# A 256-column moving operand read as interleaved 16-column runs

## The chip, the cores and the metric

One NeuronCore of a Trainium2 chip runs the kernel. The metric is the device time of one execution in microseconds (us), lower is better. A NeuronCore has five engines that run their own instruction streams and meet at semaphores: TensorE (PE in the profile; its weight loads are listed as PEld), VectorE (DVE), ScalarE (ACT), GpSimd (POOL) and SyncE (SP). Here SP and POOL only start transfers, apart from a few constants that POOL writes at the start.

## The reference

Attention of 8x8 heads over a small state, then two feed-forward blocks over 4608 tokens. The second feed-forward block is the part that the change touches.

```python
def _attn_ref(x, state):            # x (8, 8, 512, 64), state (8, 8, 32, 64)
    ...                             # two softmaxes, xread and sread
    return np.concatenate([xread, sread], axis=2)

def _moe_ref(x, w_in, w_out):       # 4608 tokens, 512 -> 2048 -> 512
    h = np.maximum(x @ w_in, 0.0)
    return h * h @ w_out

def _moe2_ref(x, w1, w2, w3, w_out):    # 4608 tokens, 512 -> 1024 -> 1024 -> 512
    a = x @ w1
    b = x @ w2
    h = a * b @ w3
    return h @ w_out

def reference(**kwargs):
    attn_out = _attn_ref(...)
    x = attn_out.transpose(0, 2, 1, 3).reshape(4608, 512)
    x = _moe_ref(x, ...)
    return _moe2_ref(x, ...)
```

## The kernel before

**Number format.** Every matrix product is made of float32r operands: each float32 value is held as a rounded high part and the rest as a low part, and a product takes three matmuls, high by high, high by low, low by high. The helper `product` (line 658) issues them. It is the helper's line 661 that the profile names for nearly every matmul. In `nc.tensor.matmul(dst, w, m)` the second argument is the stationary operand (the weights, 128 columns, loaded by a weight load of its own before each matmul), the third is the moving operand, whose columns are streamed through the array. The profile prints a matmul as `dst<-moving,stationary`.

**Stages.** Up to about 100 us, tables are built (`w3` times `moe2_w_out`, the state times `w_in`). Then follow the eight batches of 512 tokens, with attention woven in, through the first feed-forward block (matmuls with 512 moving columns), and a ninth, short block of 256 tokens (moving columns 256, from some 680 us on). At 720.92 us the second feed-forward block begins, called stage 2 here. It lasts to the end.

**Stage 2.** The products `x @ w1` and `x @ w2` are not made directly. For each pair of token tiles (halves of the 512 tokens of a batch) and the two matrices, a Strassen-Winograd scheme takes seven products of sums in place of eight. The seven sums on the side of the weights, S_hi and S_lo, lie in rows of several tensors (`E_hi`, `E_lo`, `top`, `aT_hi`, `X_hi` and others, hence the many names in the profile). The seven sums on the side of the tokens are `B_hi[:, j, kk]` and `B_lo[:, j, kk]`, j = 0 to 6, kk = 0, 1 for the two halves of the inner dimension, each 256 columns wide. They are views into the tensors `X_hi` and `X_lo`, which start `SHIFT = 80` columns (320 bytes) into them:

```python
        B_hi, B_lo = (t[:, 0:N_SETS + 1].rearrange("p k n -> p (k n)")[:, SHIFT:SHIFT + N_SETS * C]
                      .rearrange("p (j k n) -> p j k n", j=N_SETS, k=2) for t in (X_hi, X_lo))
```

In the built program every stationary operand of the kernel starts 128 bytes past a multiple of 512 bytes within its partition, and so does every moving operand, but for these block sums: they start 448 bytes past one, which is the 320 bytes of SHIFT further.

The engines' programs of stage 2 are written out by hand, in chunks. For batch t and output chunk m (0 to 7):

- `ab_chunk(t, m)` on TensorE: seven products of two halves and three passes, 42 matmuls of 256 moving columns, into four banks of `ps_h` and `ps_t`. It starts when VectorE is done with the banks of the chunk before (`ab_done`), at m = 0 it waits for each new set of token sums (`set_ready`), and the fifth product waits until ScalarE has copied the first (`P1_copied`).
- `out_chunk(t, m - 1)` on TensorE: four output tiles by three passes, 12 matmuls of 512 moving columns, from `v_hi` and `v_lo` into `ps_y`. It waits for `ab_split`.
- On VectorE and ScalarE, `ab_chunk` adds the seven products up into a and b, multiplies them (`ab_done`), rounds to `v_hi` (ScalarE) and subtracts to `v_lo` (VectorE, `ab_split`). At m = 7 both also round and subtract the seven token sums of the next batch.

TensorE alternates `ab_chunk` and `out_chunk`, 64 of each. The 256 state tokens come last: `rest_ab(m)`, 24 matmuls of 256 columns straight from `B_hi` and `B_lo` (which then hold plain tokens), and `out_chunk` with 256 columns, eight of each. So 64 x 42 + 8 x 24 = 2880 matmuls read a block sum as the moving operand. Results leave through `stage` to the output `out`, which is transposed (feature rows, token columns); the host reorders it.

Of the kernel before, what the change touches and what calls it, by code (L numbers as in the profile page):

```python
# [34 lines left out]
def build_program(nc, x_tok, x_T, state_T, moe_w_in, moe_w_out, moe2_w1, moe2_w2, w3_T, moe2_w_out, out):  # L35
    P = 128
# [17 lines left out]
    KM = DM // P  # L54
# [5 lines left out]
    KINDS = 8  # L60
# [22 lines left out]
    with ctx:  # L83
# [69 lines left out]
        def sr(a):  # L153
# [9 lines left out]
        B_hi, B_lo = (t[:, 0:N_SETS + 1].rearrange("p k n -> p (k n)")[:, SHIFT:SHIFT + N_SETS * C]  # L163
                      .rearrange("p (j k n) -> p j k n", j=N_SETS, k=2) for t in (X_hi, X_lo))
# [4 lines left out]
        T3 = B12  # L169
        B_src = (B11, T2, T3, T1, B21, T4, B22)  # L170
        sums_needed = (0, 3, 2, 1, 0, 4, 0)

        P1, c11 = t1[:, 0, 0:HT], t1[:, 0, 0:HT]
        u2, c22 = t1[:, 0, HT:TT], t1[:, 0, HT:TT]
# [4 lines left out]
        def rest_bank(m):  # L179
            return (bank_W, bank_X, bank_Y, bank_Z)[m % 4]  # L180
# [4 lines left out]
        S_hi = [[E_rows[k] for k in (0, 1, 2, 3, 8, 9, 10)], [E_rows[k] for k in (11, 4, 5, 6, 7, 12, 13)],  # L185
                [X_hi[:, 8 + j] for j in range(N_SETS)],
                [X_hi[:, 15], X_lo[:, 15], E_rows[15]] + aT_rows[0]]
# [466 lines left out]
        def _(pe):  # L654
            def passes(w_hi, w_lo, m_hi, m_lo):
                return (w_hi, m_hi), (w_hi, m_lo), (w_lo, m_hi)

            def product(dst, w_hi, w_lo, m_hi, m_lo, first, last):

                for n, (w, m) in enumerate(passes(w_hi, w_lo, m_hi, m_lo)):  # L660
                    mm = nc.tensor.matmul(dst, w, m, start=first and n == 0, stop=last and n == 2)  # L661
                return mm
# [182 lines left out]
            def ab_chunk(t, m):  # L845
                chunk = KG * t + m
                wait_for(pe, ab_done, chunk)
                if isinstance(t, int) and t == 0 and m % 4 == 0:
                    for g in (m // 2, m // 2 + 1):
                        pe.wait_ge(S_loaded[g], 16 * 2 * N_SETS)  # L850
                cols = slice(m % 4 * P, (m % 4 + 1) * P)
                for j, dst in enumerate(places):
                    if m == 0:
                        pe.wait_ge(set_ready, N_SETS * t + j + 1)
                    if j == 4:
                        pe.wait_ge(P1_copied, chunk + 1)
                    for kk in range(2):
                        g = m // 4 * 2 + kk
                        mm = product(dst, S_hi[g][j][:, cols], S_lo[g][j][:, cols], B_hi[:, j, kk], B_lo[:, j, kk],
                                     kk == 0, kk == 1)  # L860
                    mm.then_inc(prod_done, 1)

            def rest_ab(m):

                wait_for(pe, ab_done, KG * NB + max(m - 3, 0))
                if m % 4 == 0:
                    pe.wait_ge(A21_loaded[m // 4], 16 * 4)
                cols = slice(m % 4 * P, (m % 4 + 1) * P)
                bank = rest_bank(m)
                for dst, sets in ((bank[:, 0:NT], (0, 4)), (bank[:, NT:2 * NT], (1, 5))):  # L870
                    for c in range(KM):
                        if m == 0:
                            pe.wait_ge(set_ready, N_SETS * NB + c // 2 + 1)
                        g = m // 4 * 2 + c % 2
                        last = product(dst, S_hi[g][sets[c // 2]][:, cols], S_lo[g][sets[c // 2]][:, cols],
                                       B_hi[:, c // 2, c % 2], B_lo[:, c // 2, c % 2], c == 0, c == KM - 1)
                last.then_inc(rest_full, 1)

            def out_chunk(t, m, n=TT):
# [655 lines left out]
```

## Time and profile before

| | |
|---|---|
| median of 3 runs | 1259.64 us (1258.2 to 1260.02) |
| the profiled execution's own time | 1259.05 us |
| its span, first to last instruction | 1257.4 us |
| TensorE's mean granted clock | 0.992 |
| TensorE busy | 1236.8 us, 98% |
| weight loads busy | 1079.5 us, 86% |
| VectorE, ScalarE busy | 809.9 us (64%), 496.0 us (39%) |

The span is 1.65 us shorter than the execution's own time; the rest lies before the first and after the last instruction. Busy times of TensorE overlap: a row's duration runs from a matmul's start to its modelled end, while the next one starts before that end. How fast TensorE goes is therefore read from the distance of starts in the timeline, and not from durations. A row of the timeline with `x4` merges four instructions of the same kind.

### The profile page before, as it was taken

Reading aid. Unit: us, or ns where it says so; the run is one execution under the profiler, and the core shown is the slowest. Engines: PE = TensorE matmul, PEld = TensorE weight load, DVE = VectorE, ACT = ScalarE, POOL = GpSimd, SP = SyncE. Lnnn points to the kernel's source line nnn. Section 1 sums busy time; section 2 is a strip of 40 time slices with the busy share of each in tenths; the row PEclk is TensorE's granted clock in tenths of the full one; section 3 lists DMA queues with packets and bytes.
Section 4 is the critical chain, followed back from the end, with each engine's and each line's share of the span. In section 5 each row is a group of like instructions: output and inputs, shape, how many; then the busy total and the mean of one; then the engine's idle time right before and its main releaser. Section 6 shows DMA issues by size and latency. Waiting matters only on the chain.

```text
span 1257.4 us, 19633 instructions
## 1 busy us (share of the span) xinstructions
PE 1236.8 (98%) x7177; PEld 1079.5 (86%) x7177; DVE 809.9 (64%) x1445; ACT 496.0 (39%) x936; POOL 56.6 (5%) x101
## 2 busy tenths in 40 slices
PE   8988999999999999999999999999999999999998
PEld 6656888888888888888889999999999999999998
DVE  6666877678696866667544667575757575757541
ACT  6565565455555555445443422121212121212111
POOL 1000001111011100000000000000000000000000
PEclk9988999999999999999999999999999999999999
DMA  8986444344434322122112950101011010100210
GB/s 296 357 290 240 138 151 163 138 144 161 150 134 157 135 104 93 62 84 67 68 67 79 371 204 1 68 6 62 18 48 33 34 33 33 33 33 0 85 63 22
DMA packets 64632, 139.13 MB, mean 111 GB/s; under 512 B 5696, under 2 KB 6720, under 8 KB 64576
## 3 DMA queue, kind: packets, MB, share of 16 engines
q1 hardware_dynamic: 53984, 100.68, 23.5%
q0 software_dynamic: 10592, 37.75, 8.2%
q8 instruction: 29, 0.48, 0.2%
q14 instruction: 27, 0.22, 0.1%
HBM read 84.93 MB, written 53.48 MB: 110 GB/s over the span
## 4 chain that ended last, share of the span: by engine, by line
PE 96%; DMA 3%; DVE 1%; ACT 0%; issue 0%; SPq 0%; POOL 0%; DVEq 0%; POOLq 0%; ACTq 0%
PE ps_y L661 48%; PE ps_h L661 27%; PE ps_t L661 18%; DMA g_scratch<-g_extra 1%; DMA wp_scratch<-stage 1%; DMA g_scratch<-stage 1%; PE ps_t L720 1%; PE ps_h L720 0%; PE ps_t L685 0%; DMA raw<-in_moe_w_out 0%; DVE v_lo L1207 0%; ACT v_hi L951 0%; DVE t L1207 0%; DVE stage L1318 0%; DVE stage L1296 0%
## 5 line engine op out<-in xcount | busy, mean ns | idle before, releaser
L951 ACT CAST v_hi<-t 128x512 fp32r<-128x512 f32 (+1 forms) x216 | 129.0, 597 | 443.7 <-DVE t L1207 442.8
L661 PE MATMUL ps_y<-v_hi,X_hi 128*128 128x512 f32 (+1 forms) x576 | 219.6, 381 | 3.3 <-DVE stage L1296 3.3
L1207 DVE TENSOR_TENSOR v_lo<-t,v_hi 128x512 fp32r<-128x512 f32 (+1 forms) x216 | 143.0, 662 | 118.7 <-ACT v_hi L951 111.9
L661 PE MATMUL ps_y<-v_hi,X_lo 128*128 128x512 f32 (+1 forms) x576 | 218.1, 379 | 0.0
L661 PE MATMUL ps_y<-v_lo,X_hi 128*128 128x512 f32 (+1 forms) x576 | 218.1, 379 | 0.0
L1207 DVE TENSOR_TENSOR t<-t 128x256 f32<-128x256 f32 (+1 forms) x272 | 143.5, 547 | 101.8 <-ACT t L1051 99.0
L1051 ACT ACTIVATE t<-ps_h 128x512 f32<-128x512 f32 (+1 forms) x144 | 82.5, 573 | 157.4 <-PE ps_h L661 155.8
L661 PEld LDWEIGHTS ps_y<-v_hi,X_hi 128*128 128x128 f32 x576 | 108.8, 189 | 23.0 <-issue 3.7
L661 PEld LDWEIGHTS ps_y<-v_hi,X_lo 128*128 128x128 f32 x576 | 108.7, 189 | 20.4
L661 PEld LDWEIGHTS ps_y<-v_lo,X_hi 128*128 128x128 f32 x576 | 108.9, 189 | 19.5
L1207 DVE TENSOR_TENSOR t<-t,ps_t 128x256 f32<-128x256 f32 (+1 forms) x132 | 72.5, 549 | 47.4 <-PE ps_t L661 33.6
L661 PE MATMUL ps_h<-aT_hi,GA 128*128 128x512 f32 (+1 forms) x288 | 95.7, 378 | 0.5 <-ACT g_extra L951 0.5
L661 PE MATMUL ps_h<-aT_hi,GB 128*128 128x512 f32 (+1 forms) x288 | 95.7, 377 | 0.0
L661 PE MATMUL ps_y<-v_hi,GB 128*128 128x512 f32 (+1 forms) x288 | 91.6, 382 | 0.4 <-DVE v_lo L1207 0.4
L661 PE MATMUL ps_y<-v_hi,GA 128*128 128x512 f32 (+1 forms) x288 | 91.6, 381 | 0.0
L1207 DVE TENSOR_TENSOR t<-t,ps_h 128x256 f32<-128x256 f32 x132 | 54.9, 416 | 55.0 <-PE ps_h L661 42.8
L1207 DVE TENSOR_TENSOR t<-ps_t,t 128x512 f32<-128x512 f32 x64 | 44.2, 690 | 45.5 <-PE ps_t L661 44.7
L951 ACT COPY t<-ps_h 128x256 f32<-128x256 f32 (+1 forms) x74 | 31.5, 426 | 84.7 <-PE ps_h L661 80.8
L661 PEld LDWEIGHTS ps_h<-aT_hi,GA 128*128 128x128 f32 x288 | 53.3, 188 | 11.2 <-ACT g_extra L951 0.9
L661 PEld LDWEIGHTS ps_y<-v_hi,GB 128*128 128x128 f32 x288 | 53.3, 188 | 10.3 <-DVE v_lo L1207 0.6
L1207 DVE TENSOR_TENSOR X_lo<-raw,X_hi 128x512 fp32r<-128x512 f32 x66 | 45.3, 686 | 26.0 <-ACT X_hi L951 25.6
L661 PEld LDWEIGHTS ps_h<-aT_hi,GB 128*128 128x128 f32 x288 | 53.3, 188 | 10.0
(235 smaller groups left out, 2811.2 us busy)
## 6 DMA issues: line engine op xcount, KB each, us to landing
raw<-g_scratch SPq DMA_DIRECT2D x64, 256.0 KB
raw<-in_moe_w_in SPq DMA_DIRECT2D x32, 256.0 KB
raw<-in_x_T SPq DMA_DIRECT2D x32, 256.0 KB
raw<-in_x_tok SPq DMA_DIRECT2D x32, 256.0 KB
y_scratch<-stage POOLq DMA_DIRECT2D x8, 1024.0 KB, 6.2
s_scratch<-top POOLq DMA_DIRECT2D x32, 256.0 KB, 2.5
s_scratch<-E_lo POOLq DMA_DIRECT2D x32, 256.0 KB, 3.5
raw<-y_scratch SPq DMA_DIRECT2D x8, 1024.0 KB, 5.3
```

Of the source, the lines that this page charges most:

```text
L661: mm = nc.tensor.matmul(dst, w, m, start=first and n == 0, stop=last and n == 2)
L720: last = nc.tensor.matmul(pair_banks(p)[:, par, :], w[half, 0, par, rows], m[half], start=n == 0, stop=n == 2)
L951: return nc.scalar.copy(dst, src)
L1051: nc.scalar.activation(t1[:, f % 2, 0:n], ps_h[:, f % 2, 0:n], ACT.Relu).then_inc(relu_done, 1)
L1207: return nc.vector.tensor_tensor(dst, a, b, op)
```

## The change

A function `woven` is applied to the moving operand of the block products, in `ab_chunk` and in `rest_ab` of TensorE. The 256 columns of a block sum are read in another order: as two halves of 128 columns, 8 runs of 16 each, taking one run of the first half, the run of the same number of the second, and so on. The access pattern in the program goes from one run of 256 to [8 steps of 16 columns][2 steps of 128 columns][16 columns]. The columns of the result land in PSUM in that order and stay in it (everything after works column by column), so `out` holds each 256 tokens in the woven order, and the host undoes it. Nothing else differs: each engine's instructions, their order, their waits, sizes and start addresses are the same, and so are the transfers.

```diff
@@ -169,6 +169,10 @@
         T3 = B12
         B_src = (B11, T2, T3, T1, B21, T4, B22)
         sums_needed = (0, 3, 2, 1, 0, 4, 0)
+
+        def woven(t):
+
+            return t.rearrange("p (s k n) -> p k s n", s=2, n=P // KINDS)
 
         P1, c11 = t1[:, 0, 0:HT], t1[:, 0, 0:HT]
         u2, c22 = t1[:, 0, HT:TT], t1[:, 0, HT:TT]
@@ -856,8 +860,8 @@
                         pe.wait_ge(P1_copied, chunk + 1)
                     for kk in range(2):
                         g = m // 4 * 2 + kk
-                        mm = product(dst, S_hi[g][j][:, cols], S_lo[g][j][:, cols], B_hi[:, j, kk], B_lo[:, j, kk],
-                                     kk == 0, kk == 1)
+                        mm = product(dst, S_hi[g][j][:, cols], S_lo[g][j][:, cols], woven(B_hi[:, j, kk]),
+                                     woven(B_lo[:, j, kk]), kk == 0, kk == 1)
                     mm.then_inc(prod_done, 1)
 
             def rest_ab(m):
@@ -873,7 +877,8 @@
                             pe.wait_ge(set_ready, N_SETS * NB + c // 2 + 1)
                         g = m // 4 * 2 + c % 2
                         last = product(dst, S_hi[g][sets[c // 2]][:, cols], S_lo[g][sets[c // 2]][:, cols],
-                                       B_hi[:, c // 2, c % 2], B_lo[:, c // 2, c % 2], c == 0, c == KM - 1)
+                                       woven(B_hi[:, c // 2, c % 2]), woven(B_lo[:, c // 2, c % 2]),
+                                       c == 0, c == KM - 1)
                 last.then_inc(rest_full, 1)
@@ -1528,7 +1533,7 @@
-    out = r.results[0]["out"].T
+    out = r.results[0]["out"].reshape(d_out, -1, 8, 2, 16).transpose(1, 3, 2, 4, 0).reshape(-1, d_out)
```

## Rows read from the trace of the kernel before

**Rows 1.** The page: span, busy time of each engine, the chain by engine

```profile
span 1257.4 us, 19633 instructions
...
PE 1236.8 (98%) x7177; PEld 1079.5 (86%) x7177; DVE 809.9 (64%) x1445; ACT 496.0 (39%) x936; POOL 56.6 (5%) x101
...
PE 96%; DMA 3%; DVE 1%; ACT 0%; issue 0%; SPq 0%; POOL 0%; DVEq 0%; POOLq 0%; ACTq 0%
```

**Rows 2.** Busy times in one stretch, from the first to the last block product

```profile
core 0: us, PE busy (x) PEld busy (x) DVE busy (x) ACT busy (x) POOL busy (x), PEclk, DMA share, GB/s
720.92:1248.33 527.41, 527.41 (x3746) 495.07 (x3745) 320.80 (x628) 109.83 (x216) 6.78 (x9) 1.00 0.13 47
```

**Rows 3.** Timeline of TensorE, one chunk of block products

```profile
start us, us, engine line op out<-in xcount [idle before <-releaser]
906.01 0.28 PE L661 MATMUL ps_h<-X_hi,E_hi 128*128 128x256 f32 x1
906.13 0.28 PE L661 MATMUL ps_h<-X_lo,E_hi 128*128 128x256 f32 x1
...
910.84 0.28 PE L661 MATMUL ps_t<-X_hi,E_lo 128*128 128x256 f32 x1
910.96 0.40 PE L661 MATMUL ps_y<-v_hi,GB 128*128 128x512 f32 x1
```

**Rows 4.** Timeline of the 256-column matmuls of the short block, no shift

```profile
699.92 0.28 PE L661 MATMUL ps_y<-v_hi,X_lo 128*128 128x256 f32 x1
700.04 0.28 PE L661 MATMUL ps_y<-v_hi,X_hi 128*128 128x256 f32 x1
...
720.80 0.28 PE L661 MATMUL ps_y<-v_hi,X_lo 128*128 128x256 f32 x1
720.92 0.28 PE L661 MATMUL ps_h<-X_hi,E_hi 128*128 128x256 f32 x1
```

**Rows 5.** Timeline of 512-column matmuls of the first block

```profile
400.89 0.39 PE L661 MATMUL ps_y<-v_hi,X_hi 128*128 128x512 f32 x1
...
403.61 0.39 PE L661 MATMUL ps_h<-aT_hi,GA 128*128 128x512 f32 x1
```

**Rows 6.** Timeline: from 512 to 256 columns and back, no shift

```profile
601.35 0.28 PE L661 MATMUL ps_t<-x_hi,a2T_hi 128*128 128x256 f32 x1
601.46 0.28 PE L661 MATMUL ps_t<-x_lo,a2T_hi 128*128 128x256 f32 x1
...
604.10 0.28 PE L661 MATMUL ps_t<-x_hi,a2T_lo 128*128 128x256 f32 x1
604.22 0.40 PE L661 MATMUL ps_y<-v_hi,X_hi 128*128 128x512 f32 x1
604.46 0.40 PE L661 MATMUL ps_y<-v_lo,X_hi 128*128 128x512 f32 x1
```

**Rows 7.** Timeline of four 128-column transposes and their weight loads, window cut inside

```profile
588.15 0.27 PE L685 MATMUL ps_t<-ident,e 128*128 128x128 f32 x1
588.15 0.38 PE L685 MATMUL ps_t<-ident,e 128*128 128x128 f32 x2
588.15 0.49 PE L685 MATMUL ps_t<-ident,e 128*128 128x128 f32 x3
...
588.37 0.14 PEld L685 LDWEIGHTS ps_t<-ident,e 128*128 128x128 f32 x1
588.48 0.19 PEld L661 LDWEIGHTS ps_y<-v_hi,X_hi 128*128 128x128 f32 x1
```

**Rows 8.** Timeline of TensorE, an output chunk after block products

```profile
903.25 0.40 PE L661 MATMUL ps_y<-v_hi,GB 128*128 128x512 f32 x1
903.49 0.39 PE L661 MATMUL ps_y<-v_lo,GB 128*128 128x512 f32 x1
```

**Rows 9.** Timeline of VectorE and ScalarE around that output chunk, m = 7

```profile
903.67 0.68 DVE L1207 TENSOR_TENSOR t<-t,ps_t 128x512 f32<-128x512 f32 x1
904.38 0.76 DVE L1207 TENSOR_TENSOR t<-t 128x256 f32<-128x256 f32 x2
905.06 0.69 DVE L1207 TENSOR_TENSOR X_lo<-stT,X_hi 128x512 fp32r<-128x512 f32 x1
905.66 0.69 DVE L1207 TENSOR_TENSOR X_lo<-raw,X_hi 128x512 fp32r<-128x512 f32 x1
906.26 0.69 DVE L1207 TENSOR_TENSOR v_lo<-t,v_hi 128x512 fp32r<-128x512 f32 x1
906.87 0.68 DVE L1207 TENSOR_TENSOR X_lo<-sreadT,X_hi 128x512 fp32r<-128x512 f32 x1
907.47 0.69 DVE L1207 TENSOR_TENSOR X_lo<-raw,X_hi 128x512 fp32r<-128x512 f32 x1
...
906.92 0.37 ACT L951 COPY t<-ps_h 128x256 f32<-128x256 f32 x1 [1.12 <-PE ps_h L661]
```

**Rows 10.** Timeline: the last block product and the last transfer's issue

```profile
1248.21 0.28 PE L661 MATMUL ps_t<-X_hi,raw_r 128*128 128x256 f32 x1
...
1253.45 0.75 POOL L649 DMA_DIRECT2D out<-stage  x1 [30.37 <-DVE stage L1455]
```

## The prediction

> **What bounds the kernel now.** I read the page first, then the busy times by stretch, then the timeline of single matmuls. The page says that TensorE is busy 98% of the span and that the chain which ends last is TensorE's for 96% of it, with no line of another engine above 3% [rows 1]. In the stretch that the change touches TensorE is busy for all of its 527.41 us at clock 1.00, its full 2.4 GHz, while VectorE is busy for 320.80 us and ScalarE for 109.83 us [rows 2]. Nobody is waited for there, so each nanosecond between the starts of two matmuls goes into the time. The time after the last block product, 9.2 us to the span's end, holds other work [rows 1, 10].
>
> What sets the distance between two starts? A chunk of 42 block products takes 910.96 - 906.01 = 4.95 us, 117.9 ns each [rows 3]. The short block before also has 256 moving columns, but operands without the shift: 174 matmuls start in 720.92 - 700.04 = 20.88 us, 120.0 ns each [rows 4]. Matmuls of 512 columns, also without the shift, take 2.72 us for 12, 226.7 ns each [rows 5]. The difference of the last two, 106.7 ns, is what 256 columns cost (2.4 a nanosecond). So a matmul pays 13.3 ns on top of its columns, whatever its width, and a block product pays 11.2 ns. What differs between [rows 3] and [rows 4] is where the moving operand starts relative to the stationary one, 320 bytes against 0, modulo 512 bytes. I take that as the cause of the 2.1 ns: part of the surcharge is the two reads of SBUF, the moving columns and the next matmul's weights, meeting in the same place.
>
> That the weight load takes part shows in two more places. Four transposes of 128 columns would stream in 53 ns each, but the merged rows of one, two and three end 0.11 us apart, and the next two weight loads start 0.11 us apart: the pace is the weight load's own, 0.22 us for two, so 105 to 115 ns [rows 7]. And where 256-column matmuls follow 512-column ones, the first distance is 0.11 us and the mean over the 24 is 2.87 / 24 = 119.6 ns; the first one's successor had its weights loaded in advance, the others did not [rows 6]. So a 256-column stream runs at the weight load's pace of about 109 ns plus what the two reads cost each other.
>
> **The change, part by part.** No instruction is added, removed or moved, on any engine or queue. What changes is the order in which 2880 matmuls read their moving columns, and the order of columns in PSUM and in the output; VectorE, ScalarE and the transfers handle the columns as before, at no cost, since the sizes and the contiguous patterns on their side are the same.
>
> The read order matters as follows. A contiguous moving read covers 1024 bytes of each partition in the 107 ns of its 256 columns; the weight load beside it covers its 128 columns, 512 bytes, in about the same time [rows 7]. Modulo 512 bytes the faster read laps the slower one, whatever the start, and a shift only chooses when they meet. The woven read covers the same 512-byte range once, 16 columns (64 bytes) from the first half and the 16 at the same place of the second, 512 bytes further. Modulo 512 bytes it advances at just the weight load's rate, and it starts 320 bytes ahead. The two never meet, if places repeat every 512 bytes or a power of two below that and down to about 128 bytes.
>
> The price of a matmul without the meeting is shown by no row. Its bounds are 106.7 ns, the columns alone [rows 4, 5], and 117.9 ns, no gain [rows 3]. The nearest row is the weight load's pace, 105 to 115 ns [rows 7]; I take 109.0 ns, a little under its middle, since a stream of plain weight loads has nothing else to pay. Each matmul saves 8.9 ns, and 2880 save 25.6 us. All of it lies on the path. The sum against the profiled execution is 1259.05 - 25.6 = 1233.5 us. The median of the runs stands 0.6 us above that execution, so I forecast 1234.0 us.
>
> A small term I cost at nothing: an output chunk after block products takes 906.01 - 903.25 = 2.76 us against 2.72 us in the first block [rows 3, 5, 8], and the same slow first matmul of 0.24 us follows the unshifted run [rows 6]. The weight loads come out of a 256-column stream late and catch up. If they came out on time, 64 times 0.04 us, 2.6 us more, would go; I keep that for the range.
>
> Is there cover for 25.6 us on the other engines? The tightest place is m = 7, where VectorE also makes the token sums. It ends the last multiplication at 904.38 + 0.76 = 905.14 [rows 9], and TensorE starts the next chunk, which waits for it, at 906.01 [rows 3]: 0.87 us in hand. A chunk gets 42 x 8.9 ns = 0.37 us shorter; even if VectorE, back to back there, gained nothing, 0.50 us are left. The last token sum is ready at 907.47 + 0.69 = 908.16, and its product starts 36 matmuls into the chunk, at 910.25, then some 0.7 us earlier: 1.4 us in hand. `v_lo` is ready at 906.95 and is wanted at 910.96, then 0.7 us earlier. ScalarE's copy of the first product ends at 907.29 [rows 9]; the fifth product wants it at 908.84. Late next would be VectorE at m = 7, from about 20 ns less per matmul on, which no case here reaches.
>
> **The rivals.**
>
> *Half the gain.* The places are finer or coarser than I assume, or the weight load is not as even as the woven read, and they still meet for part of the time. The nearest row is the first distance of [rows 6], 0.11 us on the clock of the timeline; I price it halfway, at 113.4 ns: 4.5 ns x 2880 = 13.0 us less, 1246.6 us.
>
> *Nothing moves.* The surcharge belongs to the hand-over from one matmul to the next (new weights, new bank) or to issuing two instructions per matmul, and the 2.1 ns between [rows 3] and [rows 4] come from something else than the place of the reads. For it: 13.3 ns is the same for 256 and 512 columns, which suits a fixed hand-over. Against it: nothing but the addresses is systematically different between those two groups. Time: 1259.6 us. The Trainium skill, "TensorE: Matmul & The Clock Gate", Part 2, says that the moving operand and the weights have separate read ports and that loading the next weights takes no read bandwidth from the running matmul; by that rule the read order could change nothing, 1259.6 us. The trace's 2.1 ns speak against it, weakly.
>
> *The lock holds them together.* Two reads that advance at one rate either never meet or always do. If the weight load runs 320 bytes off from where I place it, because it starts earlier or later in the matmul, the woven read keeps the conflict for the whole matmul. I price it as the loss of what the shift brings, 120.0 ns [rows 4]: 2.1 ns x 2880 = 6.0 us more, 1265.6 us.
>
> *A jump costs time (the other side).* The woven read has 16 runs and so 15 jumps of the address; the kernel before has no moving operand with a jump, so no row prices it. Place: inside each of the 2880 matmuls. Below, a jump costs nothing; above, not more than a whole change of matmul, 13.3 ns [rows 4, 5], which would make 306 ns and some 540 us more. It decides from (117.9 - 106.7) / 15 = 0.75 ns on, for below that it hides in the distance of today. At the time of four columns, 1.67 ns, a matmul takes 106.7 + 25.0 = 131.7 ns, 39.7 us more: 1299.4 us. For it: each run is just 16 columns. Against it: the read of a run has 6.7 ns in which the next address can be worked out. The Trainium skill, "SBUF — State Buffer", Specifications, says that reads need two hits on a 16-byte line for full rate; a run of 16 columns has four on each of its lines, so by that rule a jump is free. No row here shows it.
>
> **How the numbers follow.** Full gain 0.37 (1234.0), half gain 0.18 (1246.6), nothing 0.18 (1259.6), held together 0.09 (1265.6), jump 0.18 (1299.4). A difference of 0.2%, 2.5 us, is about what a measurement of this kernel can tell from none; it takes 0.9 ns per block product. So faster 0.55, same 0.18, slower 0.27. The range takes in all cases but the jump: from 1229 us (108 ns per matmul, with at least 1 ns left on top of the columns, and the 2.6 us of the output chunks) to 1268 us. The likeliest case alone reaches from 1229 to 1240 us.
>
> **What would show it.** Right: the 42 starts of a chunk span 4.58 us (109.0 ns), the mean batch of stage 2 falls by 3.0 us, everything before 720.9 us stays, TensorE remains without idle time in stage 2 and VectorE's busy time with it. Half: 4.76 us. Nothing: 4.95 us. Held together: 5.04 us. Jump: 5.5 us or more, with longer rows of the single matmul, since the stream itself would be slower. I would be wrong altogether if TensorE got idle time at the start of chunks, which would mean that VectorE is the bound at m = 7.

## The result, and the profile after

The changed kernel takes 1265.2 us (median of 6 runs, 1264.84 to 1265.45) against 1259.3 us for the kernel before (median of 6): ratio 1.0048, 95% interval 1.0035 to 1.0061. It is 0.5% slower, where the forecast said 2% faster.

The page of the changed kernel, span, busy times and the chain by engine, to be held against [rows 1]:

```profile
span 1263.8 us, 19633 instructions
...
PE 1243.0 (98%) x7177; PEld 1085.7 (86%) x7177; DVE 809.9 (64%) x1445; ACT 496.4 (39%) x936; POOL 56.6 (4%) x101
...
PE 96%; DMA 3%; DVE 1%; ACT 0%; issue 0%; SPq 0%; POOL 0%; DVEq 0%; POOLq 0%; ACTq 0%
```

Busy times of the changed kernel from the first to the last block product, as [rows 2]:

```profile
core 0: us, PE busy (x) PEld busy (x) DVE busy (x) ACT busy (x) POOL busy (x), PEclk, DMA share, GB/s
720.85:1254.54 533.69, 533.69 (x3745) 500.94 (x3744) 320.83 (x628) 109.94 (x216) 6.78 (x9) 1.00 0.13 46
```

The timeline of TensorE in the changed kernel, the start of an output chunk and one chunk of block products, as [rows 3, 8]:

```profile
start us, us, engine line op out<-in xcount [idle before <-releaser]
928.84 0.39 PE L665 MATMUL ps_y<-v_hi,GA 128*128 128x512 f32 x1
929.07 0.40 PE L665 MATMUL ps_y<-v_lo,GA 128*128 128x512 f32 x1
...
939.40 0.28 PE L665 MATMUL ps_h<-X_hi 128*128 128x256 f32 x1
939.52 0.28 PE L665 MATMUL ps_h<-X_lo,X_hi 128*128 128x256 f32 x1
...
944.44 0.39 PE L665 MATMUL ps_y<-v_hi,GA 128*128 128x512 f32 x1
```

Stage 2 starts where it did (720.85 us, before 720.92), its clock is 1.00, VectorE and ScalarE do the same work in the same time, and TensorE is busy throughout. The stretch has grown from 527.41 to 533.69 us. A chunk of 42 block products now takes 944.44 - 939.40 = 5.04 us (5.036 before rounding), 119.9 ns from start to start, against 117.9 ns. The typical chunk of the trace takes 5.036 us against 4.950 us, and the output chunk behind it 2.764 against 2.757 us: 64 x 0.093 = 6.0 us. The eight chunks of the state tokens add 0.4 us. That is the whole 6.4 us by which the span grew.

### The profile page after: what moved, and what is told of

Read it like the earlier page. It is cut to its first block, busy times and chain, and to the rows that moved or that the text cites. A ratio compares the mean times of both kernels' runs of the same rounds, so it can differ in the third digit from the quotient of the medians.

```text
span 1263.8 us, 19633 instructions
## 1 busy us (share of the span) xinstructions
PE 1243.0 (98%) x7177; PEld 1085.7 (86%) x7177; DVE 809.9 (64%) x1445; ACT 496.4 (39%) x936; POOL 56.6 (4%) x101
## 4 chain that ended last, share of the span: by engine, by line
PE 96%; DMA 3%; DVE 1%; ACT 0%; issue 0%; SPq 0%; POOL 0%; DVEq 0%; POOLq 0%; ACTq 0%
PE ps_y L665 48%; PE ps_h L665 27%; PE ps_t L665 19%; DMA g_scratch<-g_extra 1%; DMA wp_scratch<-stage 1%; DMA g_scratch<-stage 1%; PE ps_t L724 1%; PE ps_h L724 0%; PE ps_t L689 0%; DMA raw<-in_moe_w_out 0%; DVE v_lo L1212 0%; ACT v_hi L956 0%; DVE t L1212 0%; DVE stage L1323 0%; DVE stage L1301 0%
```

## The experiments

Most runs use one method: TensorE issues eight block chunks (m = 0 to 7) per batch, and each may read in its own way, so that one run measures seven ways side by side. A table names the read; values that differ from the true ones change no step of the program. Each of these runs was executed once. "Distance" below is the mean from start to start over the last 36 matmuls of a chunk, from the trace; within a run the eight batches agree to 0.2 ns, and m = 0 and 7 of every such run gave the 117.8 ns (or 120.0 ns, woven) of their kernel again. (The mean over a whole chunk differs from it by 0.1 to 0.5 ns, since the first few distances are others.)

```diff
+            def flat_row(t, j, kk, shift, n=256):
+                at = shift + (2 * j + kk) * P * 2
+                return t[:, 0:N_SETS + 1].rearrange("p k n -> p (k n)")[:, at:at + n]
+            def plain(shift=SHIFT):
+                return lambda t, j, kk: flat_row(t, j, kk, shift)
+            def woven(n=16, s=2, shift=SHIFT):
+                return lambda t, j, kk: flat_row(t, j, kk, shift).rearrange("p (s k n) -> p k s n", s=s, n=n)
...
+                        read = READ.get(m, READ[None])
+                        mm = product(dst, S_hi[g][j][:, cols], S_lo[g][j][:, cols], read(X_hi, j, kk),
+                                     read(X_lo, j, kk), kk == 0, kk == 1)
```

A "place" below is 16 columns, 64 bytes; places are counted from the weights' start. All weights start in the same kind of place, so these runs alone can't tell whether it is the distance from the weights that counts or the address of the moving operand itself.

### Does the start matter, and is there a start that keeps the woven read clear?

```diff
+            READ = {None: plain(), 1: plain(0), 2: plain(16), 3: plain(32), 4: plain(48), 5: plain(64), 6: plain(112)}
```

> The kernel before (contiguous reads), but in chunks m = 1 to 6 of every batch the block sums are read from another start: shift 0, 16, 32, 48, 64 and 112 columns in place of 80 (m = 0 and 7 keep 80). The values read are then partly those of a neighbouring sum, so a and b are other numbers there. Theory 'meeting' (the moving read and the next weight load cost each other something when they come to the same place modulo 512 bytes): shift 0 gives 120.0 ns per matmul as in the short block, shift 80 117.9 ns, and the others differ among each other by a ns or more. Theory 'hand-over' (the address has no part): 117.9 ns in all of them.

```diff
+            READ = {None: woven(), 1: woven(shift=0), 2: woven(shift=16), 3: woven(shift=32), 4: woven(shift=48), 5: woven(shift=64), 6: woven(shift=112)}
```

> The changed read order in every chunk, and in chunks m = 1 to 6 the same other starts as in the run with contiguous reads: shift 0, 16, 32, 48, 64, 112 columns (values partly those of a neighbouring sum). Theory 'held together' (woven read and weight load advance at one rate, so they meet throughout or never): strong dependence on the shift, one or more of them near 109 ns, others at 120 ns or above. Theory 'jump' (15 jumps of the address cost 2.1 ns together): 2.1 ns above the contiguous read at each shift. Theory 'ceiling' (any other order than the contiguous one at shift 80 gives the 120.0 ns of the unshifted): 120 ns in all.

Measured, in ns:

| shift, columns | 0 | 16 | 32 | 48 | 64 | 80 | 112 |
|---|---|---|---|---|---|---|---|
| contiguous | 120.0 | 117.8 | 120.0 | 117.8 | 120.0 | 117.8 | 117.8 |
| woven | 120.0 | 120.0 | 120.0 | 120.0 | 120.0 | 120.0 | 120.0 |

Two chunks of the contiguous run, m = 3 (shift 32) and m = 4 (shift 48), with the output chunk behind each:

```profile
928.66 0.28 PE L661 MATMUL ps_h<-X_hi,E_hi 128*128 128x256 f32 x1
...
933.70 0.39 PE L661 MATMUL ps_y<-v_hi,GA 128*128 128x512 f32 x1
...
936.46 0.28 PE L661 MATMUL ps_h<-X_hi 128*128 128x256 f32 x1
...
941.41 0.39 PE L661 MATMUL ps_y<-v_hi,GA 128*128 128x512 f32 x1
```

5.04 against 4.95 us, and 16 columns further on is the only difference in the moving read. So the address does matter, with a fine grain: a start an odd number of places away from the weights' is worth 2.2 ns, an even number nothing. "Hand-over" as the whole story is out. But the woven read has no start at all at which it is clear: neither "never meet" nor "always meet" describes seven equal results. Of the three theories for the woven read only "ceiling", 120 ns in all, came true.

### Is it the jumps?

```diff
+            READ = {None: plain(), 1: woven(4), 2: woven(8), 3: woven(16), 4: woven(32), 5: woven(64), 6: woven(16, 4)}
```

> At shift 80, chunks m = 1 to 5 read woven runs of 4, 8, 16, 32 and 64 columns, m = 6 four quarters of 64 columns in turn, 16 columns each; m = 0 and 7 contiguous. Only a permutation of columns that differs by chunk, so the output's columns are mixed. Theory 'jump': the surcharge over 117.9 ns goes with the number of jumps: 63, 31, 15, 7, 3 and 15 jumps, so about +9, +4.3, +2.1, +1, +0.4 and +2.1 ns. Theory 'held together': runs of 4 to 32 columns all advance at the weight load's rate and give 120 ns alike, and the quarters, which advance at half that rate, differ from them.

Measured: 126.7, 123.3, 120.0, 118.6 and 117.8 ns for runs of 4, 8, 16, 32 and 64; 118.6 ns for the quarters. The first row looks like a price per jump. The quarters speak against it: 15 jumps like the change, about a third of its surcharge over 117.8 ns. "Held together" is out as well, since runs of 4 to 32 are far from alike.

### Taking the weights' reads away

`still(n, shift)` repeats n columns until there are 256, `one_weight` gives all 128 weights the same column (step 0), `far_weights` puts 128 columns of `E_hi`, 32 apart, in place of the weights, `odd_woven` puts the second half 144 columns off, and `split` reads all places of one kind, then all of the other. These runs compute other numbers in a and b.

```diff
+            def one_weight(t):
+                return t[:, 0:1].to_broadcast([P, P])
...
+            def far_weights(t):
+                return E_hi.rearrange("p k (c n) -> p (k c) n", n=32)[:, :, 0]
```

With `one_weight` the weight load is still there, 128 columns long; what goes is the spread of its addresses.

```diff
+            READ = {None: plain(), 1: still(16, 0), 2: still(16, 32), 3: still(16, 64), 4: still(16, 96), 5: still(64, 64), 6: still(128, 0)}
```

> Moving operands that stay in one place: m = 1 to 4 read the same 16 columns sixteen times, at shift 0, 32, 64 and 96; m = 5 the same 64 columns four times at shift 64; m = 6 the same 128 columns twice at shift 0; m = 0 and 7 contiguous at shift 80. Products are then of repeated columns, so a and b are other numbers. Theory 'meeting': the weight load passes the 64 bytes only once in its 512, so the distance falls towards 109 ns, about alike for the four places. Theory 'hand-over': 117.9 to 120.0 ns whatever is read. Theory 'jump': jumps backwards cost as those forward, 120 ns for 15 of them, less for 3 and 1.

Measured: 122.2, 121.7, 122.2, 121.7 ns for 16 repeated columns; 120.0 ns for 64 at shift 64 and for 128 at shift 0, as contiguous reads at these starts. Staying in one place, which I took for the way to be out of the weight load's way, is 3.9 to 4.4 ns slower than the contiguous read at 80. No theory had forecast that.

```diff
+            READ = {None: plain(), 1: still(16, 16), 2: still(16, 0), 3: odd_woven(0), 4: odd_woven(16), 5: split(0), 6: split(1)}
+            WEIGHTS = {1: one_weight, 2: one_weight}
```

> Reads arranged by bit 6 of the address (64-byte places, two kinds: 'even' and 'odd'; the earlier runs gave 117.8 ns to contiguous reads whose start differs from the weights' by an odd number of places, 120.0 ns to an even one). Chunks m = 1 and 2: all 128 weights are one column of an even place (step 0), the moving read repeats 16 columns of an odd (m = 1) or even (m = 2) place. m = 3 and 4: woven read with the second half 144 columns away, so kinds run 0, 11, 00, 11 ... at even and odd start. m = 5 and 6: contiguous weights, the moving read takes all 8 places of one kind, then all 8 of the other (m = 5 even first, m = 6 odd first). Values are partly those of other columns. Theory 'two banks' (a weight load and a moving read in the same kind of place stall each other): m = 1 near 109 ns, m = 2 clearly slower, m = 3 and 4 apart from one another by some ns or one of them below 117 ns. Theory 'fixed' (about 117.8 ns is the hand-over, and only the last 2.2 ns and what lies above depend on places): m = 1 and 2 both at 117.8 ns or above.

Measured: 122.2, 121.1, 120.0, 121.4, 120.0, 120.0 ns. Weights of one column and a moving read in the other kind of place, which by "two banks" cannot collide, took 122.2 ns: that theory, in its simple form, fell. "Fixed", 117.8 ns or above for both, held here and fell in the next run.

```diff
+            READ = {None: plain(), 1: still(16, 16), 2: still(16, 0), 3: plain(), 4: still(4, 0), 5: still(4, 16), 6: still(4, 0)}
+            WEIGHTS = {1: far_weights, 2: far_weights, 3: one_weight, 6: one_weight}
```

> Chunks m = 1 and 2: the 128 weights are taken 32 columns apart (each from a new 16-byte piece, all in even places), the moving read repeats 16 columns of an odd (m = 1) or even (m = 2) place. m = 3: one weight column, contiguous moving read at shift 80. m = 4 and 5: contiguous weights, moving read repeats 4 columns of an even or odd place. m = 6: one weight column and 4 moving columns. Other numbers in a and b there. Theory 'two banks': m = 1 near 109 ns, m = 2 the slowest of all, m = 3 between. Theory 'fixed': none below 117.8 ns. If the number of 16-byte pieces read decides, m = 3 and m = 6 are the fastest.

Measured: 216.6 and 229.8 ns for weights 32 columns apart; 113.3 ns for one weight column with the contiguous read; 111.7 ns three times for 4 repeated columns, whatever the weights. The chunk with one weight column (m = 3):

```profile
961.15 0.28 PE L661 MATMUL ps_h<-X_hi,E_hi 128*128 128x256 f32 x1
...
965.92 0.39 PE L661 MATMUL ps_y<-v_hi,GA 128*128 128x512 f32 x1
```

4.78 us, 4.4 ns per matmul less than with the kernel's own weights at the same moving addresses. So at this start the contiguous read's distance depends on which addresses the weight load reads. That this is a toll which the weights' reads always take is not shown: the last runs below reach the same 113.3 ns with the kernel's own weights from another start.

The 4 repeated columns are the fastest read of all, although they never leave one place. With the weights 32 columns apart the weight load itself is long. Its rows before and in chunk m = 1, at the end of that chunk, and in m = 3 (one weight column):

```profile
936.65 0.19 PEld L661 LDWEIGHTS ps_y<-v_hi,GB 128*128 128x128 f32 x1
936.87 0.30 PEld L661 LDWEIGHTS ps_h<-X_hi,E_hi 128*128 128x128 f32 x1
...
945.75 0.31 PEld L661 LDWEIGHTS ps_t<-X_hi,E_hi 128*128 128x128 f32 x1
...
961.85 0.19 PEld L661 LDWEIGHTS ps_h<-X_lo,E_hi 128*128 128x128 f32 x1
```

The load lasts 0.30 to 0.33 us in place of 0.19 us, so the 216.6 and 229.8 ns are most likely its pace and no toll on the matmul; only the 13.2 ns between the two rows tell of the moving read's place.

```diff
+            WEIGHTS = {5: 64, 6: 64}
...
+                        rows = WEIGHTS.get(m, P)
+                        moved = read(X_hi, j, kk)
+                        width = {1: 128, 2: 160, 3: 192, 4: 224}.get(m, 256)
```

> Parts of the product are left out: m = 1 to 4 stream 128, 160, 192 and 224 columns instead of 256; m = 5 and 6 load 64 weight columns instead of 128, m = 5 with the contiguous read, m = 6 with the woven one; all at shift 80. Theory 'weight load is the pace' (a 256-column stream runs at the weight load's own pace, lengthened by the moving read): 128 to 224 columns take nearly what 256 take, 108 to 117 ns, and 64 weights with 256 columns fall to 109 ns or so with little difference between contiguous and woven. Theory 'hand-over': the distance falls by 13.3 ns for each 32 columns, and half the weights still give 117.9 ns contiguous and 120.0 ns woven.

Measured: 111.7 ns for each of 128, 160, 192 and 224 columns. This is a floor that doesn't depend on the columns streamed; I take it for the pace of a weight load of 128 columns, but no run loads fewer weights beside so few columns, so a fixed cost of each pair of weight load and matmul is not excluded. With half the weights: contiguous 116.7 ns, woven 120.0 ns, where "weight load is the pace" asked for about 109 ns in both. So a 256-column stream is not at the weight load's pace, as the forecast had it; the moving read sets the distance, and the woven one does not care how much the weight load reads.

### The moving read alone

`skip(n)` reads 16 columns of every n.

```diff
+            READ = {None: plain(), 1: woven(16), 2: woven(8), 3: woven(32), 4: skip(48), 5: skip(32), 6: plain(0)}
+            WEIGHTS = {m: one_weight for m in range(1, 7)}
```

> In chunks m = 1 to 6 all 128 weights are one column (step 0), which took the weight load's reads out of the way in the earlier runs: a contiguous moving read at shift 80 gave 113.3 ns there, 16 repeated columns 121 to 122 ns. Now with such weights: m = 1 woven in runs of 16, m = 2 runs of 8, m = 3 runs of 32, m = 4 runs of 16 every 48 columns, m = 5 runs of 16 every 32 columns (all at shift 80), m = 6 contiguous at shift 0. Other numbers in a and b there. Theory 'dwell' (the moving read itself is slowed when it stays in one kind of 64-byte place for more than 16 columns; jumps are free): m = 1 and 2 near 120 ns, m = 5 121 to 122 ns, m = 3, 4 and 6 113.3 ns. Theory 'jump': m = 1, 4 and 5 alike and above 113.3 ns by the same amount, m = 2 twice that, m = 3 half. Theory 'meeting' (weights and moving read cost each other): all 113.3 ns.

Measured: woven 120.0 (runs of 16), 120.1 (8), 117.8 (32); every 48 columns 117.9, every 32 columns 120.0; contiguous at shift 0 116.7 ns. The woven chunk (m = 1) of this run:

```profile
914.51 0.28 PE L661 MATMUL ps_h<-X_hi,E_hi 128*128 128x256 f32 x1
...
919.55 0.40 PE L661 MATMUL ps_y<-v_hi,GA 128*128 128x512 f32 x1
```

5.04 us, as in the changed kernel, with a single column for all weights. This decides the main point: the contiguous read goes from 117.8 to 113.3 ns when all weights are one column, the woven read stays at 120.0 ns. Its time is its own and doesn't hang on what the weight load reads. "Meeting" (113.3 ns in all) is out, and "dwell" missed too: it gave 113.3 ns to m = 3, 4 and 6, which took 117.8, 117.9 and 116.7 ns. The last of these is a contiguous read at an even start, 3.4 ns above the odd one, so the kind of start counts with one weight column as well.

```diff
+            READ = {None: plain(), 1: skip(48), 2: skip(32), 3: skip(48, 0), 4: skip(80), 5: still(32), 6: woven(64, shift=0)}
```

> With the kernel's own weights: runs of 16 columns taken every 48 columns (m = 1 at shift 80, m = 3 at shift 0), every 32 columns (m = 2, shift 80), every 80 columns (m = 4, shift 80); m = 5 the same 32 columns eight times at shift 80; m = 6 woven runs of 64 at shift 0. Values are those of neighbouring sums. Steps of 48 and 80 have 15 jumps as the change has, but alternate between even and odd places as the contiguous read does; steps of 32 have 15 jumps and stay in one kind. Theory 'dwell': 117.8 ns for m = 1, 4 and 5, 120.0 ns for m = 3 and 6, 121 to 122 ns for m = 2. Theory 'jump': 120.0 ns or more for m = 1, 2 and 4 alike, and m = 5 between.

Measured: 120.0, 122.2, 120.0, 117.8, 120.0, 120.0 ns. Two chunks of it, m = 4 (16 columns of every 80) and m = 5 (32 columns, eight times):

```profile
938.83 0.28 PE L661 MATMUL ps_h<-X_hi 128*128 128x256 f32 x1
...
943.78 0.40 PE L661 MATMUL ps_y<-v_hi,GA 128*128 128x512 f32 x1
...
946.53 0.28 PE L661 MATMUL ps_h<-X_hi 128*128 128x256 f32 x1
...
951.58 0.39 PE L661 MATMUL ps_y<-v_hi,GB 128*128 128x512 f32 x1
```

Fifteen jumps cost nothing (4.95 us), seven cost 2.2 ns (5.05 us). "Jump" is out. "Dwell" failed too: it gave 117.8 ns to m = 1 and 5, which took 120.0. What the two steps of 80 and 48 columns differ in is this: 80 columns are five places, which modulo four is one place ahead, as in the contiguous read; 48 are three, which modulo four is one back.

`pairs(n)` is the woven read with the second half n columns away.

```diff
+            READ = {None: plain(), 1: pairs(160), 2: pairs(192), 3: pairs(144), 4: pairs(160, 32, 32), 5: pairs(176), 6: pairs(160, shift=64)}
```

> Woven runs of 16 with the second half further away than 128 columns, at the kernel's own weights (values of a neighbouring sum in part): m = 1 160 columns, m = 2 192, m = 3 144, m = 4 runs of 32 at 160, m = 5 176, all at shift 80; m = 6 160 at shift 64. In places modulo four they go 1 3 2 0 3 1 0 2 (160), 1 1 2 2 3 3 0 0 (192, as the change), 1 2 2 3 3 0 0 1 (144), 1 0 2 1 3 2 0 3 (176). Theory 'two places': what counts is odd or even alone, so 160 and 192 both give 120.0 ns as the change. Theory 'four places': 192 gives 120.0 ns, 160 and 176, which never stay in a place, give 117.8 to 118.6 ns, 144 121.4 ns as at shift 16.

Measured: 122.8, 120.0, 121.4, 120.0, 120.0, 120.0 ns. A miss for "four places" as I had put it: not to stay in a place isn't enough, 160 columns came out slowest of the six; 192 and 144 columns took what it gave them. "Two places" gives 160 and 192 the same at one start and is out.

```diff
+            READ = {None: plain(), 1: pairs(160), 2: skip(80), 3: still(32), 4: still(64), 5: plain(16), 6: woven(shift=0)}
+            WEIGHTS = {m: one_weight for m in range(1, 7)}
```

> All weights from one column of an even place: m = 1 woven runs of 16 with the halves 160 columns apart, m = 2 runs of 16 every 80 columns, m = 3 32 columns repeated eight times, m = 4 64 columns repeated four times (all shift 80), m = 5 contiguous at shift 16, m = 6 woven at shift 0. Theory 'four places': m = 2 and 4 give the 113.3 ns of the contiguous read at 80, m = 3 more (117 to 118 ns). Theory 'two places': m = 3 too gives 113.3 ns. In both m = 5 tells whether 16 is like 80 (113.3 ns) or like 0 (116.7 ns), and m = 6 stays at 120.0 ns.

Measured: 122.2, 113.3, 120.0, 113.3, 113.3, 120.1 ns. Two chunks of it, m = 3 (32 columns repeated) and m = 4 (64 repeated):

```profile
929.30 0.28 PE L661 MATMUL ps_h<-X_hi,E_hi 128*128 128x256 f32 x1
...
934.34 0.39 PE L661 MATMUL ps_y<-v_hi,GA 128*128 128x512 f32 x1
...
937.06 0.28 PE L661 MATMUL ps_h<-X_hi 128*128 128x256 f32 x1
...
941.84 0.39 PE L661 MATMUL ps_y<-v_hi,GA 128*128 128x512 f32 x1
```

4.78 us for four places over and over, 5.04 us for two. "Four places" had the sides right, though it gave m = 3 only 117 to 118 ns. Every read with one weight column and an odd start that went through the places modulo four in rising order, jump or no jump (contiguous, 64 repeated, 16 of every 80), took 113.3 ns; every read of whole places in another order took 117.8 to 122.2 ns. The 4 repeated columns, a quarter of a place, stand outside this with their 111.7 ns.

### Whole kernels

The change with runs of 64, so that the order modulo four is the contiguous one:

```diff
-            return t.rearrange("p (s k n) -> p k s n", s=2, n=P // KINDS)
+            return t.rearrange("p (s k n) -> p k s n", s=2, n=64)
...
-    out = r.results[0]["out"].reshape(d_out, -1, 8, 2, 16).transpose(1, 3, 2, 4, 0).reshape(-1, d_out)
+    out = r.results[0]["out"].reshape(d_out, -1, 2, 2, 64).transpose(1, 3, 2, 4, 0).reshape(-1, d_out)
```

> The change with runs of 64 columns in place of 16 (4 runs, 3 jumps; a correct kernel with its output laid out to match). Theory 'order of places': modulo four 64-byte places the read goes 1, 2, 3, 0 throughout as the contiguous one does, so 117.8 ns and the time of the kernel before, within 0.1%. If weaving as such costs, about 1265 us.

1259.24 us, ratio to the kernel before 1.0003 (0.9994 to 1.0012): weaving as such is free, and every chunk has 117.8 ns.

An odd number of places for the 512-column matmuls of the first block too:

```diff
+        sb("pad", [P, 16])
         aT_hi = sb("aT_hi", [P, 2, HG, S], F32R)
...
-        sb("line", [P, 48])
+        sb("line", [P, 32])
```

> Contiguous reads in all, a correct kernel. A pad of 16 columns before aT_hi moves aT, t, v, stage, stT, bd and sreadT up by 64 bytes, so that 3072 + 288 of the 512-column matmuls read their moving operand an odd number of 64-byte places from the weights instead of an even one; 616 of the 2880 block products, whose weights lie in the moved tensors, go the other way, 480 short ones gain. If the 2.2 ns of odd against even at 256 columns also holds at 512 and whatever the tensors: (3360 + 480 - 616) x 2.2 ns = 7.1 us less than the kernel before, about 1252.3 us. If it is a matter of the 256-column streams alone: (616 - 480) x 2.2 ns = 0.3 us more, no difference.

1265.21 us, ratio 1.0045 (1.0031 to 1.0059), slower: a plain miss. Stage 2 begins at 728.05 us in place of 720.92, and from 100 us to there the usual distance of 512-column matmuls (those of 200 to 300 ns) rose from a mean of 227.1 to 229.8 ns. In the first block an odd start takes at 512 columns what it gives at 256. The output chunks of stage 2, whose `v_hi` and `v_lo` moved too, did not get longer (2.753 against 2.759 us on average).

The run shows something else. 616 block products now have weights one place nearer or further, and by the rule of odd and even distance they should cost 2.2 ns more each, 0.02 us in a chunk. The chunks took 4.948 us against 4.950 us. So the distance from the weights is not borne out as the thing that counts; the moving operand's own address would fit as well, and no run here tells them apart in a whole chunk.

The start that had the fastest output chunk in the first run of shifts:

```diff
-    SHIFT = 80
+    SHIFT = 112
```

> Contiguous reads, SHIFT = 112 in place of 80 (448 bytes from the weights' place in place of 320), a correct kernel. In the run of shifts a chunk at 112 took 4947 ns and the output chunk behind it 2720 ns, against 4950 and 2757 ns at 80: 64 x 40 ns = 2.5 us less, 0.2%, if it adds up over the kernel. Otherwise no difference.

1255.26 us, ratio 0.9977 (0.9968 to 0.9986). The output chunks took 2.720 us in place of 2.757 us, 2.4 us in all. Of the remaining 1.4 us some 0.9 us came from something new. The first chunks of stage 2, m = 1 and m = 2 of the first batch:

```profile
728.32 0.29 PE L661 MATMUL ps_h<-X_hi,E_hi 128*128 128x256 f32 x1
...
733.10 0.39 PE L661 MATMUL ps_y<-v_hi,GA 128*128 128x512 f32 x1
...
735.83 0.28 PE L661 MATMUL ps_h<-X_hi,E_hi 128*128 128x256 f32 x1
...
740.78 0.39 PE L661 MATMUL ps_y<-v_hi,GA 128*128 128x512 f32 x1
```

4.78 and 4.95 us, with the same addresses and the kernel's own weights: 113.3 and 117.8 ns. The fast one stands behind 24 matmuls of 256 columns, the slow one behind 512-column ones. Eight block chunks in all are fast, m = 0 and 1 of the first batch and six of the eight of the state tokens, all behind 256-column output chunks; in the kernel before, at SHIFT = 80, the chunks at the same places take 117.8 ns. So I halved some matmuls of the output chunks, in the kernel with SHIFT = 112:

```diff
+            HALVED = (0, 1, 3, 6, 12, 2, 0, 3)
...
+                    operands = passes(w_hi[:, cols], w_lo[:, cols], v_hi[:, m % 2, 0:n], v_lo[:, m % 2, 0:n])
+                    for k, (w, moved) in enumerate(operands):
+                        halves = 2 if n == TT and 3 * o + k >= 12 - HALVED[m] else 1
+                        for h in range(halves):
+                            part = slice(h * n // halves, (h + 1) * n // halves)
+                            last = nc.tensor.matmul(ps_y[:, o, part], w, moved[:, part], start=m == 0 and k == 0,
+                                                    stop=m == KG - 1 and k == 2 and h == halves - 1)
```

> The kernel with SHIFT = 112, and in the output chunks the last 1, 3, 6, 12 and 2 matmuls (m = 1, 2, 3, 4, 5; m = 7 also 3; m = 0 and 6 none) are issued as two of 256 columns each, a correct kernel. Output chunk m comes before block chunk m + 2. Theory 'state' (a chunk settles at 113.3 or 117.8 ns by how the weight loads stand to the moving reads when it begins, and a stretch of 256-column matmuls before it sets this): some of the block chunks 3 to 7 and 1 settle at 113.3 ns, most likely those behind 6 and 12 halved ones. A halved matmul costs 2 x 120.0 - 226.7 = 13 ns, a chunk at 113.3 ns saves 42 x 4.4 = 187 ns. Theory 'place' (only the very first chunks differ, for a reason of their own): all settle at 117.8 ns and the kernel is 27 x 13 ns x 8 = 2.8 us slower than with SHIFT = 112 alone, 1258.1 us.

1251.1 us, ratio to the kernel before 0.9935 (0.9918 to 0.9952). From the second batch on, the chunks behind 1, 2, 3, 6 and 12 halved matmuls all settle at 113.3 ns, those behind none (m = 2 and m = 0) at 117.8 ns. One halved matmul is enough, and "place" is out. Then one in each output chunk:

```diff
+            HALVED = (1,) * KG
```

> SHIFT = 112, contiguous reads, and in each output chunk only the last matmul as two of 256 columns; a correct kernel. If every block chunk settles at 113.3 ns: a chunk 4.78 us and its output chunk 2.74 us, 7.52 us in place of 7.71 us, 64 times 0.19 us = 12 us less than the kernel before: about 1247 us.

1246.21 us, ratio 0.9899 (0.9883 to 0.9916): 1.0% faster than the kernel before, 1.5% faster than the changed one. A chunk (m = 4) of it, ahead of its output chunk:

```profile
929.44 0.29 PE L661 MATMUL ps_h<-X_hi 128*128 128x256 f32 x1
929.56 0.28 PE L661 MATMUL ps_h<-X_lo,X_hi 128*128 128x256 f32 x1
...
934.22 0.39 PE L894 MATMUL ps_y<-v_hi,GA 128*128 128x512 f32 x1
```

4.78 us; with its output chunk 7.52 us in place of 7.71 us, as forecast. The output chunk takes 2.741 us where it took 2.720 us, so a halved matmul costs 21 ns here and not 13. The same edit on the kernel before (SHIFT = 80) and on the changed kernel:

> The kernel before (SHIFT = 80) with the same single halved matmul per output chunk; a correct kernel. If the state is open to any start an odd number of places away: 113.3 ns and about 1247 to 1249 us. If it needs SHIFT = 112: 117.8 ns and 64 x 13 ns = 0.8 us more than the kernel before.

> The changed kernel (woven, SHIFT = 80) with the same single halved matmul per output chunk; a correct kernel. If the woven order itself sets its pace, as it did with one weight column: still 120.0 ns in every chunk, 1265 to 1266 us. If its 120.0 ns is only the slower of two states: below 118 ns and less than 1260 us.

1259.57 us, ratio 1.0002 (0.9992 to 1.0011), and 1267.24 us, ratio 1.0066 (1.0049 to 1.0083). At SHIFT = 80 every chunk stays at 117.8 ns and the woven read stays at 120.0 ns, a little above its forecast because the chunk and its output chunk grew by 0.03 us together. The 113.3 ns are open to the contiguous read from the one start and were not reached in the other two. The woven read at SHIFT = 112 with a halved matmul was not run, so a shorter distance of it is not excluded there.

## Why the prediction was wrong

**What bounds the kernel** was right. TensorE is busy for all of stage 2 in both kernels, no chunk begins with a wait, nothing before stage 2 moved, and the cover on VectorE was never asked for. The 2880 matmuls and the way a distance turns into time were right: about 2.0 ns x 2880 and 0.5 us of output chunks give the 6.4 us.

**The address has a part.** Right, and finer than the 2.1 ns of [rows 3, 4] could tell: it goes by odd and even places of 64 bytes, 117.8 and 120.0 ns at seven starts. That the cause is the two reads meeting in one place is not shown; the 3.4 ns between odd and even starts with one weight column and the run with the pad speak against it.

**"So a 256-column stream runs at the weight load's pace of about 109 ns plus what the two reads cost each other."** Wrong in both halves. What can be the weight load's pace in this stream is 111.7 ns, the floor measured with 128 to 224 columns; I had taken the transposes' 105 to 115 ns [rows 7] and its middle. And the stream is held by the moving read: with half the weights it still takes 116.7 ns, with one weight column 113.3 ns.

**"The price of a matmul without the meeting ... I take 109.0 ns."** This is the term that failed: 109.0 ns was forecast, 119.9 ns measured. The step under it is "Modulo 512 bytes it advances at just the weight load's rate ... The two never meet." I had asked only what the two reads do to each other, and had no price for what the moving read does to itself. Giving the weight load a single column takes 4.4 ns from the contiguous read and nothing from the woven one: 120.0 ns is what that order takes by itself. The bound "no gain" that I gave as the upper end of this term was no bound, since the traces before contain only contiguous reads.

**"Held together"** gave the right number, 1265.6 us, for the wrong reason, by luck. It priced a conflict with the weight load by the unshifted rows. The two 120.0 ns are alike in size, but the woven one depends on no start (seven of them) and on no weights (128, 64 or one column), so it isn't a meeting that is held. (The 113.4 ns of "half the gain" was likewise only a midpoint; that a contiguous read reached 113.3 ns later doesn't bear it out.)

**"A jump costs time"** is refuted: 16 columns of every 80, with 15 jumps, take 117.8 ns with the kernel's weights and 113.3 ns with one column, just as the contiguous read. Here the Trainium skill, "SBUF — State Buffer", Specifications (at least two hits on a 16-byte line for full rate), agrees with this 117.8 ns as to jumps, but its rule does not give the 120.0 ns of runs of 16, with four hits on each line.

**"Nothing moves"** is refuted too: the read order alone made 1259.3 us into 1265.2 us, and 64 bytes of start make 2.2 ns. The Trainium skill, "TensorE: Matmul & The Clock Gate", Part 2, says that loading the next weights takes nothing from the running matmul; the traces do not bear that out at SHIFT = 80, where the contiguous read took 117.8 ns with 128 weight columns, 116.7 ns with 64 and 113.3 ns with one column repeated. At SHIFT = 112 it took 113.3 ns with all 128, so there the loading costs no more than that of one column.

**The likely cause**, as far as the runs carry it, is the order in which the moving read passes from one 64-byte place to another. Modulo four places (256 bytes) the contiguous read goes in rising order, and the change visits each kind twice in a row (1 1 2 2 3 3 0 0). With one weight column, every other order of whole places cost 4.5 to 8.9 ns more than the rising one from an odd start, and a rising read from an even start 3.4 ns more. That the places repeat every four is suggested by 64 against 32 repeated columns and by steps of 80 against 48. That the surcharge is the order's own is shown; that rising order is the rule is argued from a handful of orders, and three results don't fit it. The 4 repeated columns never leave a place and took 111.7 ns, the least of all. The quarters stay in each place four times in a row (1 1 1 1 2 2 2 2 ...) and cost 0.8 ns, less than the change. And runs of 4 and 8 visit the places as runs of 16 do, but took 126.7 and 123.3 ns with the kernel's weights (runs of 8 with one weight column 120.1 ns). What in the memory or in TensorE does this stays open, as does why 512-column matmuls of the first block prefer an even start, and what makes the state of 113.3 ns reachable from SHIFT = 112 and not from 80.

## What to carry to other kernels

Keep a moving operand's columns contiguous, or in runs of 64 float32 columns, which was free here with halves 128 columns apart; if they must be interleaved more finely, measure it, since an order without a single added instruction cost 2.0 ns on each of 2880 matmuls. When a cost is put down to two parties, price each of them alone before the sum is made: one chunk with a single weight column would have told that the woven read takes 120.0 ns by itself. And where a loop has several equal chunks, give each its own variant; one run then shows six variants beside the original, from start to start, to a tenth of a nanosecond.

## What was not expected of the hardware

- A stream of 256-column matmuls with identical addresses has two stable distances, 117.8 and 113.3 ns. From SHIFT = 112 one matmul of 512 columns issued as two of 256 ahead of a chunk switches to the faster one within its first few matmuls, and some 20 ns buy 0.17 us.
- With weights taken 32 columns apart 256-column matmuls start every 216.6 ns (moving read in an odd place) or 229.8 ns (even place); the weight load's own rows grow from 0.19 to over 0.30 us.
- A 256-column moving read that repeats 4 columns takes 111.7 ns, 6.1 ns less than the contiguous one at SHIFT = 80, with the kernel's weights as with one column.
- Starts that differ by 64 bytes change a 256-column matmul by 2.2 ns one way and a 512-column one of the first block by 2.7 ns the other way.
